# Attention units by head: scores, transposes and values of one head together, values ahead of the hidden-layer tile

## The chip, the cores and the metric

The program runs on one core of one Trainium2 chip. The metric is device time in microseconds of one execution. Engines named below: TensorE (PE in the profile; PEld are its weight loads), VectorE (DVE), ScalarE (ACT), GpSimd (POOL) and SyncE (SP), which issues most of the DMAs.

## The reference

Three stages follow each other. The attention stage has 2 batches, 8 heads, 576 positions and head size 64; half of the heads see the last 32 positions only, the other half see every 32nd position. A mixture of 8 experts over all 1152 rows comes next, and then a mixture in which each row takes its two best experts.

```python
scores = scale * np.matmul(q, k.transpose(0, 1, 3, 2))
mask_local = (rel >= 0) & (rel < stride)
mask_strided = (rel >= 0) & (pos[None, :] % stride == pos[:, None] % stride)
scores = np.where(masks[None, :, :, :], scores, -1000000000.0)
attn = np.exp(scores - np.max(scores, axis=-1, keepdims=True))
attn = attn / (np.sum(attn, axis=-1, keepdims=True) + 1e-09)
x = np.matmul(attn, v)            # rearranged to 1152 x 512
# first mixture: P from x @ w_gate (8 rounds of row and column sums)
for e in range(E):
    out += P[:, e:e + 1] * (np.maximum(x @ w1[e], 0.0) @ w2[e])
# second mixture: the same products, each row with its two best experts only
```

## The kernel before, in words

The change touches the attention stage alone. Its work is cut into 16 units U (`UNITS`); two units make a pair of heads (`g = U // 2`). Units 0 to 3 and 8 to 11 are local (tiles of 96 queries by 128 keys, three per head), units 4 to 7 and 12 to 15 are strided (72 by 72, four per head). In each unit both heads of a pair are worked on: head h=0 has its 64 rows of `qT` and `kT` on partitions 0 to 63, head h=1 on partitions 64 to 127.

There is no scheduler: each engine runs the order written in its block, and semaphores join them. For one unit U the steps are:

- TensorE, `scores(U)` (L1060, L1069): for both heads one matmul that puts the mask into PSUM, then the score matmuls, tile by tile with the two heads taking turns. The mask matmul of head h waits for the exponentials of unit U-1, head h.
- TensorE, `transpose_probs(U - 1, h)` (L1082): the probabilities of the unit before, 0 then 1, each after GpSimd has scaled them (`prs_ready`).
- TensorE, `transpose_half` (L1046): transposes of q or k of the next pair, up to unit 13.
- TensorE, `keep_warm` (L1185): matmuls on zeros without use of their result, one to three a unit in units 3 to 8.
- TensorE, `fill(f)` (L1137 to L1139), units 10 to 15: twelve matmuls of one hidden tile of the first mixture, ahead of `values(U - 1)`. It waits until ScalarE and VectorE have emptied the tile before (`hhi_ready`, `hlo_ready`).
- TensorE, `values(U - 1)` (L1100 local, L1106 strided): probabilities times v, into output partitions 0 to 63 for the one head and 64 to 127 for the other. It waits for both copies of the transposed probabilities (`pT_act` by ScalarE, `pT_dve` by VectorE). After unit 9 the gate logits of batch 0 follow (L1115, L1116).
- VectorE: row maxima of both heads (L764), `hidden_lo` (L745), `x_lo` (L736), `probs_T` (L732), then per head the sum's reciprocal (L780, L781) with q or k copies (L724, L716) and weight splits (L741) behind head 0.
- ScalarE: `x_hi` (L560), `hidden_fill` (L578), `probs_T` (L556), the exponentials (L570), a q copy (L548), weight splits (L505).
- GpSimd: the scaling of the probabilities (L431).

## Time and profile before

| what | us |
|---|---|
| median of 3 executions | 1200.23 |
| the three executions | 1194.28, 1200.35, 1200.23 |
| the profiled execution, its own time | 1194.28 |
| its span in the profile | 1192.5 |
| attention stage in the span (to the last `values`) | 0 to about 104 |
| TensorE busy, whole span | 1165.0 (98%) |

The profile is of the fastest of the three executions. What lies around the span is 1.8 us. The page gives the TensorE clock that was granted in tenths of full speed for 40 slices of the span; its two levels are 2.4 GHz (1.00) and 1.2 GHz (0.50). In the table of stretches further down each row is one unit, cut where its first mask matmul starts. A float32 matmul stands in the trace as two records (16 records for the 8 score matmuls of a strided unit), a transpose or a matmul of the mixtures as one.

### The profile page before, as it was taken

The numbers are of one execution on the slowest core, as the hardware profiler recorded it, in microseconds if no ns is written. First come the engines' busy times: TensorE is split into PE (matmuls) and PEld (weight loads), VectorE is DVE, ScalarE is ACT, GpSimd is POOL, SyncE is SP. The second block draws the span as 40 slices with busy tenths as digits, with TensorE's granted clock in tenths as the row PEclk, the third lists the DMA queues.
The fourth block names the chain that finished last, engine by engine and source line by source line (L and its number), as shares of the span: only waits on it lengthen the run. The fifth ranks groups of instructions, "written<-read, shape, count | busy, mean of one in ns | idle before, by whom it ended". The sixth has DMA issues, their size and how long they took to land.

```text
span 1192.5 us, 19152 instructions
## 1 busy us (share of the span) xinstructions
PE 1165.0 (98%) x6697; PEld 1036.7 (87%) x6697; DVE 486.9 (41%) x1003; ACT 325.2 (27%) x710; POOL 106.7 (9%) x118
## 2 busy tenths in 40 slices
PE   7999999999999999999999999999997999999997
PEld 4677999999999999999999999999896889888885
DVE  4656524213323322411322332241136566665663
ACT  4763113102112211301211221231132334343332
POOL 3222000000000000000000000000001222222221
PEclk9689999999999999999999999999998999999999
DMA  7635104002201200400220220040003666556653
GB/s 167 153 111 163 50 1 137 5 0 70 70 0 57 84 0 0 141 0 0 70 70 0 69 72 0 0 142 27 27 18 103 183 187 178 160 155 166 164 154 79
DMA packets 82337, 96.42 MB, mean 81 GB/s; under 512 B 22176, under 2 KB 56992, under 8 KB 82304
## 3 DMA queue, kind: packets, MB, share of 16 engines
q1 hardware_dynamic: 76400, 81.23, 22.7%
q0 software_dynamic: 5904, 14.75, 5.8%
q8 instruction: 20, 0.33, 0.1%
q14 instruction: 13, 0.11, 0.0%
HBM read 85.05 MB, written 10.91 MB: 80 GB/s over the span
## 4 chain that ended last, share of the span: by engine, by line
PE 95%; DVE 1%; ACT 1%; issue 1%; SPq 1%; DMA 1%; POOL 0%; POOLq 0%; ACTq 0%; DVEq 0%
PE bank L1151 15%; PE bank L1137 15%; PE bank L1153 15%; PE bank L1152 15%; PE bank L1139 14%; PE bank L1138 14%; PE bank L1069 1%; PE bank L1082 1%; PE bank L1358 1%; ACT prs L570 1%; PE bank L1280 1%; PE bank L1060 1%; PE bank L1046 1%; PE bank L1343 1%; PE bank L1185 0%
## 5 line engine op out<-in xcount | busy, mean ns | idle before, releaser
L1151 PE MATMUL bank<-w2hi,hhi 128*128 128x512 f32 (+1 forms) x768 | 301.0, 392 | 0.0
L1153 PE MATMUL bank<-w2hi,hlo 128*128 128x512 f32 (+1 forms) x768 | 299.9, 390 | 0.0
L1152 PE MATMUL bank<-w2lo,hhi 128*128 128x512 f32 (+1 forms) x768 | 299.7, 390 | 0.0
L1137 PE MATMUL bank<-xhi,w1hi 128*128 (+1 forms) x768 | 257.9, 336 | 2.9 <-issue 2.6
L647 ACT ACTIVATE hhi<-bank 128x384 fp32r<-128x384 f32 x184 | 90.5, 492 | 611.8 <-PE bank L1139 611.8
L1139 PE MATMUL bank<-xhi,w1lo 128*128 (+1 forms) x768 | 257.0, 335 | 0.0
L1138 PE MATMUL bank<-xlo,w1hi 128*128 (+1 forms) x768 | 256.8, 334 | 0.0
L745 DVE SCALAR_TENSOR_TENSOR hlo<-bank,hhi 128x384 fp32r<-128x384 f32 (+1 forms) x256 | 139.0, 543 | 265.7 <-ACT hhi L647 234.3
L1153 PEld LDWEIGHTS bank<-w2hi,hlo 128*128 128x128 f32 (+1 forms) x768 | 141.6, 184 | 33.1
L1152 PEld LDWEIGHTS bank<-w2lo,hhi 128*128 128x128 f32 (+1 forms) x768 | 141.7, 184 | 31.0
L1151 PEld LDWEIGHTS bank<-w2hi,hhi 128*128 128x128 f32 (+1 forms) x768 | 141.7, 185 | 30.9
L844 DVE SCALAR_TENSOR_TENSOR acc<-bank,prob,acc 128x512 f32<-128x512 f32 x63 | 47.3, 751 | 266.4 <-PE bank L1153 266.4
L1137 PEld LDWEIGHTS bank<-xhi,w1hi 128*128 128x128 f32 x768 | 144.2, 188 | 4.6 <-issue 3.2
L1138 PEld LDWEIGHTS bank<-xlo,w1hi 128*128 128x128 f32 x768 | 144.2, 188 | 0.9
L1139 PEld LDWEIGHTS bank<-xhi,w1lo 128*128 128x128 f32 x768 | 144.2, 188 | 0.0
L741 DVE TENSOR_TENSOR w2lo<-w2raw,w2hi 128x1024 fp32r<-128x1024 f32 x64 | 78.1, 1221 | 13.7 <-ACT w2hi L505 13.7
L1137 PE MATMUL bank<-x2hi,w1hi 128*128 128x336 f32 x256 | 82.4, 322 | 0.9 <-ACT x2hi L680 0.9
L741 DVE TENSOR_TENSOR w1lo<-w1raw,w1hi 128x1024 fp32r<-128x1024 f32 x68 | 79.9, 1226 | 6.7 <-ACT w1hi L505 6.7
L1139 PE MATMUL bank<-x2hi,w1lo 128*128 128x336 f32 x256 | 81.7, 319 | 0.0
L1138 PE MATMUL bank<-x2lo,w1hi 128*128 128x336 f32 x256 | 81.7, 319 | 0.0
L459 POOL IOTA iotaS<- 128x336 f16 x1 | 0.4, 416 | 749.8 <-PE bank L1139 749.8
L505 ACT ACTIVATE w2hi<-w2raw 128x1024 fp32r<-128x1024 f32 x64 | 67.5, 1054 | 0.0
(176 smaller groups left out, 852.1 us busy)
## 6 DMA issues: line engine op xcount, KB each, us to landing
w1raw<-in_moe_w_dram SPq DMA_DIRECT2D x68, 512.0 KB, 4.6
w2raw<-in_moe_w_dram SPq DMA_DIRECT2D x68, 512.0 KB, 4.3
qkraw<-in_q_dram SPq DMA_DIRECT2D x16, 144.0 KB
qkraw<-in_k_dram SPq DMA_DIRECT2D x16, 144.0 KB
out_dram<-ysb POOLq DMA_DIRECT2D x3, 768.0 KB, 6.4
x1rows<-acc SPq DMA_DIRECT2D x9, 256.0 KB, 2.0
vloc<-in_v_dram SPq DMA_DIRECT2D x8, 144.0 KB
vstr<-in_v_dram SPq DMA_DIRECT2D x8, 144.0 KB
```

Source lines behind the costliest of these rows:

```text
L505: act.activation(hi, raw, ACT.Copy).then_inc(sem_out, 1)
L570: ins = act.activation(prs[0:rows, U % 2, h, t * w:(t + 1) * w], psS[h][0:rows, t * w:(t + 1) * w], ACT.Exp, bias=nmax[0:rows, h, t:t + 1] ...
L647: act.activation(hhi[:, f, :], psH[f % 4][:, 0:GT], ACT.Relu).then_inc(hhi_ready, 1)
L741: dve.tensor_tensor(lo, raw, hi.bitcast(F32), ALU.subtract).then_inc(sem_out, 1)
L745: dve.scalar_tensor_tensor(hlo[:, f, 0:n], bank[:, 0:n], 0.0, hhi[:, f, 0:n].bitcast(F32), ALU.max, ALU.subtract).then_inc(hlo_ready, 1)
L844: dve.scalar_tensor_tensor(acc[:, i, :], psY[i % TT][:, :], w, acc[:, i, :], ALU.mult, ALU.add).then_inc(acc_ready, 1)
L1137: pe.matmul(bank[:, 0:n], wh, xh(c), start=(c == 0), stop=False)
L1138: pe.matmul(bank[:, 0:n], wh, xl(c), start=False, stop=False)
L1139: ins = pe.matmul(bank[:, 0:n], wl, xh(c), start=False, stop=(c == DC - 1))
L1151: pe.matmul(psY[tt][0:rows, :], hh, w2hi[:, f, :], start=(f == 0), stop=False)
L1152: pe.matmul(psY[tt][0:rows, :], hh, w2lo[:, f, :], start=False, stop=False)
L1153: ins = pe.matmul(psY[tt][0:rows, :], hl, w2hi[:, f, :], start=False, stop=(f == FC - 1))
```

## The change

TensorE's `scores` takes the head as an argument: mask and all score matmuls of head 0, then the transposes of head 0 of the unit before, then the same for head 1. In `values` the heads no longer take turns: all tiles of head 0 after a wait for ScalarE's copy, then all of head 1 after a wait for VectorE's. In the strided units the output half is `t // 2`, so there it changes every two matmuls. `values(U - 1)` now stands ahead of `fill(f)`, and the gate logits of batch 0 stay behind the values of their unit. On VectorE `hidden_lo` goes behind `x_lo` and `probs_T`. Nothing changes on ScalarE, GpSimd and SyncE, and no instruction is added or removed.

```diff
--- before.py
+++ after.py
@@ -765,13 +765,13 @@
                                       negate=True).then_inc(max_ready, 1)
                 if U == FILL:
                     sum_parts(0, 0, WHOLE)
-                if U > FILL:
-                    f = U - FILL - 1
-                    hidden_lo(f + 1, f, psF[f])
                 if U >= 2:
                     x_lo(U - 2)
                 if U:
                     probs_T(U - 1)
+                if U > FILL:
+                    f = U - FILL - 1
+                    hidden_lo(f + 1, f, psF[f])
                 for h in range(2):
                     dve.wait_ge(exp_ready, 2 * U + h + 1)
                     if U >= 2:
@@ -1047,31 +1047,28 @@
                                        qkraw[g % 2][:, n, (4 * half + t) * P:(4 * half + t + 1) * P], ident[0:SP_ROWS, 0:SP_ROWS])
                 ins.then_inc(qk_transposed, 1)
 
-            def scores(U):
+            def scores(U, h):
                 g, c, half = U // 2, (U // 2) % PAIRS, U % 2
                 rows, tiles, w = unit_shape(U)
-                pe.wait_ge(qT_act, g + 1)
-                pe.wait_ge(qT_dve, g + 1)
-                pe.wait_ge(kT_ready, 2 * g + 2)
+                if h == 0:
+                    pe.wait_ge(qT_act, g + 1)
+                    pe.wait_ge(qT_dve, g + 1)
+                    pe.wait_ge(kT_ready, 2 * g + 2)
+                if U:
+                    pe.wait_ge(exp_ready, 2 * (U - 1) + h + 1)
                 m = mask_l[:, half, :, :] if c < LOCAL_PAIRS else spread(mask_s[:, :], 1, 4)
-                for h in range(2):
-                    if U:
-                        pe.wait_ge(exp_ready, 2 * (U - 1) + h + 1)
-                    pe.matmul(by(psS[h][0:rows], w, tiles * w), identb[0:rows, 0:rows], m, start=True, stop=False)
+                pe.matmul(by(psS[h][0:rows], w, tiles * w), identb[0:rows, 0:rows], m, start=True, stop=False)
                 for t in range(tiles):
-                    for h in range(2):
-                        if c < LOCAL_PAIRS:
-                            key = query = (half * tiles + t) * rows
-                        else:
-                            head, step, _ = strided_tile(half, h, t)
-                            query = (head * SP_T + step) // 2 * rows
-                            key = STRIDE + query
-                        ins = pe.matmul(psS[h][0:rows, t * w:(t + 1) * w],
-                                        qT[g % 2][h * DH:(h + 1) * DH, query:query + rows],
-                                        kT[g % 2][h * DH:(h + 1) * DH, key:key + w],
-                                        start=False, stop=(t == tiles - 1))
-                        if t == tiles - 1:
-                            ins.then_inc(scores_ready, 1)
+                    if c < LOCAL_PAIRS:
+                        key = query = (half * tiles + t) * rows
+                    else:
+                        head, step, _ = strided_tile(half, h, t)
+                        query = (head * SP_T + step) // 2 * rows
+                        key = STRIDE + query
+                    ins = pe.matmul(psS[h][0:rows, t * w:(t + 1) * w],
+                                    qT[g % 2][h * DH:(h + 1) * DH, query:query + rows],
+                                    kT[g % 2][h * DH:(h + 1) * DH, key:key + w], start=False, stop=(t == tiles - 1))
+                ins.then_inc(scores_ready, 1)
 
             def transpose_probs(U, h):
                 rows, tiles, w = unit_shape(U)
@@ -1092,19 +1089,15 @@
 
                     n_v = sum(6 if j % PAIRS < LOCAL_PAIRS else 2 for j in range(g % 2, g + 1, 2))
                     pe.wait_ge(v_in[g % 2], 16 * n_v)
-                pe.wait_ge(pT_act, U + 1)
-                pe.wait_ge(pT_dve, U + 1)
-                if c < LOCAL_PAIRS:
+                for h in range(2):
+                    pe.wait_ge((pT_act, pT_dve)[h], U + 1)
                     for t in range(tiles):
-                        for h in range(2):
-                            ins = pe.matmul(psO[h * DH:(h + 1) * DH, t * rows:(t + 1) * rows],
-                                            vloc[g % 2][:, h, half * tiles + t, :],
-                                            pT[0:w, h, t * rows:(t + 1) * rows], start=True, stop=True)
-                else:
-                    for h, t in ((0, 0), (1, 2), (0, 1), (1, 3), (1, 0), (0, 2), (1, 1), (0, 3)):
-                        head, step, to = strided_tile(half, h, t)
-                        ins = pe.matmul(psO[head * DH:(head + 1) * DH, to * rows:(to + 1) * rows],
-                                        vstr[g % 2][:, head, step, :],
+                        if c < LOCAL_PAIRS:
+                            head, to, vv = h, t, vloc[g % 2][:, h, half * tiles + t, :]
+                        else:
+                            head, step, to = strided_tile(half, h, t)
+                            vv = vstr[g % 2][:, head, step, :]
+                        ins = pe.matmul(psO[head * DH:(head + 1) * DH, to * rows:(to + 1) * rows], vv,
                                         pT[0:w, h, t * rows:(t + 1) * rows], start=True, stop=True)
                 ins.then_inc(heads_done, 1)
 
@@ -1202,10 +1195,10 @@
                 g = U // 2
                 if U == 2 * LOCAL_PAIRS:
                     pe.wait_ge(mask_s_ready, 1)
-                scores(U)
-                if U:
-                    transpose_probs(U - 1, 0)
-                    transpose_probs(U - 1, 1)
+                for h in range(2):
+                    scores(U, h)
+                    if U:
+                        transpose_probs(U - 1, h)
                 if g + 1 < ALLPAIRS:
 
                     transpose_half(g + 1, U % 2, 0)
@@ -1217,6 +1210,15 @@
                     keep_warm(WARM_FIRST)
                 if WARM_FROM <= U < FILL - 1:
                     keep_warm(WARM_LOCAL if g % PAIRS < LOCAL_PAIRS else WARM_STRIDED)
+                if U:
+                    values(U - 1)
+                if U == FILL - 1:
+
+                    pe.wait_ge(xlo_ready, UNITS // 2)
+                    pe.wait_ge(wgT_zeroed, 1)
+                    pe.wait_ge(wghi_ready, 1)
+                    pe.wait_ge(wglo_ready, 1)
+                    logits(psF[0], 0, WHOLE * P)
                 if U >= FILL:
                     f = U - FILL
 
@@ -1226,15 +1228,6 @@
                     else:
                         pe.wait_ge(lg_copied, 1)
                     fill(f)
-                if U:
-                    values(U - 1)
-                if U == FILL - 1:
-
-                    pe.wait_ge(xlo_ready, UNITS // 2)
-                    pe.wait_ge(wgT_zeroed, 1)
-                    pe.wait_ge(wghi_ready, 1)
-                    pe.wait_ge(wglo_ready, 1)
-                    logits(psF[0], 0, WHOLE * P)
             for h in range(2):
                 transpose_probs(UNITS - 1, h)
             fill(FILLED)
```

TensorE before, from the last hidden-tile matmul of unit 12 to the first of unit 13 (a strided unit; `bank` is PSUM, `vloc` and `vstr` are v):

```order
L1139 MATMUL bank<-xhi,w1lo 128x384
L1100 MATMUL bank<-pT,vloc_93 64x96 x6
L1060 MATMUL bank<-mask_s,identb 72x288 x2
L1069 MATMUL bank<-kT_98,qT_96 72x72 x8
L1082 MATMUL bank<-ident,prs 72x72 x8
L1046 MATMUL bank<-ident,qkraw_91 128x72 x8
L1137 MATMUL bank<-xhi,w1hi 128x384
```

The same place in the changed kernel:

```order
L1132 MATMUL bank<-xhi,w1lo 128x384
L1060 MATMUL bank<-mask_s,identb 72x288
L1068 MATMUL bank<-kT_98,qT_96 72x72 x4
L1079 MATMUL bank<-ident,prs 72x72 x4
L1060 MATMUL bank<-mask_s,identb 72x288
L1068 MATMUL bank<-kT_98,qT_96 72x72 x4
L1079 MATMUL bank<-ident,prs 72x72 x4
L1046 MATMUL bank<-ident,qkraw_91 128x72 x8
L1100 MATMUL bank<-pT,vstr_94 64x72 x8
L1130 MATMUL bank<-xhi,w1hi 128x384
```

The eight score matmuls and eight transposes of a strided unit became two blocks of four and four, and the values moved from behind the twelve hidden-tile matmuls to ahead of them.

VectorE before, at the start of unit 13:

```order
L764 TENSOR_REDUCE nmax<-bank 72x4 x2
L745 SCALAR_TENSOR_TENSOR hlo<-bank,hhi 128x384
L736 TENSOR_TENSOR xlo<-bank,xhi 128x288
L732 COPY pT<-bank 72x288
L780 TENSOR_SCALAR rinv<-rsum 72x4
```

VectorE in the changed kernel, same place:

```order
L764 TENSOR_REDUCE nmax<-bank 72x4 x2
L736 TENSOR_TENSOR xlo<-bank,xhi 128x288
L732 COPY pT<-bank 72x288
L745 SCALAR_TENSOR_TENSOR hlo<-bank,hhi 128x384
L780 TENSOR_SCALAR rinv<-rsum 72x4
```

The rest of the hidden tile moved behind the copy of the transposed probabilities.

## Rows read from the trace of the kernel before

**Rows 1.** The page, the TensorE clock granted in 40 slices.

```profile
PEclk9689999999999999999999999999998999999999
```

**Rows 2.** Busy time by unit: start:end, length, engines (count), clock, DMA share, GB/s.

```profile
20.45:24.34 3.89, 3.12 (x40) 2.45 (x40) 2.36 (x7) 2.13 (x12) 0.96 (x2) 1.00 0.93 296
29.20:33.57 4.37, 3.77 (x48) 2.60 (x48) 2.44 (x10) 2.85 (x18) 1.49 (x2) 1.00 0.88 165
33.57:37.96 4.39, 3.46 (x52) 2.57 (x53) 3.19 (x11) 4.39 (x21) 1.32 (x2) 1.00 0.95 246
37.96:44.04 6.08, 5.48 (x54) 3.76 (x54) 5.17 (x13) 5.59 (x21) 1.50 (x3) 0.63 0.74 169
44.04:50.41 6.37, 6.37 (x56) 4.55 (x55) 3.95 (x9) 4.44 (x19) 1.15 (x2) 0.50 0.45 81
50.41:56.33 5.92, 5.92 (x49) 4.40 (x48) 3.98 (x11) 3.61 (x16) 1.49 (x2) 0.50 0.51 171
56.33:65.63 9.30, 9.25 (x51) 7.10 (x49) 4.91 (x14) 4.54 (x18) 2.47 (x3) 0.50 0.66 165
65.63:72.31 6.68, 6.36 (x58) 5.11 (x57) 3.38 (x10) 4.32 (x16) 1.54 (x2) 0.91 0.00 1
83.63:89.08 5.45, 5.17 (x63) 4.43 (x64) 3.42 (x11) 3.64 (x20) 1.38 (x3) 1.00 0.66 205
```

**Rows 3.** TensorE in order of time: start, length, line; units 12 to 14.

```profile
82.91 0.72 PE L1100 MATMUL bank<-pT,vloc 128*64 128x96 f32 x12
83.56 0.44 PE L1060 MATMUL bank<-mask_s,identb 72*72 72x288 bf16 x2
83.92 0.74 PE L1069 MATMUL bank<-kT,qT 64*72 64x72 f32 x16
84.60 0.69 PE L1082 MATMUL bank<-ident,prs 72*72 72x72 f32 x8
85.13 0.67 PE L1046 MATMUL bank<-ident,qkraw 72*128 72x72 f32 x8
86.08 0.41 PE L1137 MATMUL bank<-xhi,w1hi 128*128 128x384 f32 x1 [0.28 <-issue]
...
88.36 0.72 PE L1106 MATMUL bank<-pT,vstr 72*64 72x72 f32 x16
...
91.53 0.41 PE L1137 MATMUL bank<-xhi,w1hi 128*128 128x384 f32 x1 [0.79 <-issue]
```

**Rows 4.** TensorE in order of time, one lone float32 matmul at full clock.

```profile
114.00 0.34 PE L1161 MATMUL bank<-prob,ones 128*128 128x72 f32 x2
114.14 0.48 PE L1151 MATMUL bank<-w2hi,hhi 128*128 128x512 f32 x1
```

**Rows 5.** TensorE in order of time, a local unit at full clock.

```profile
72.70 0.90 PE L1069 MATMUL bank<-kT,qT 64*96 64x128 f32 x12
73.53 0.71 PE L1082 MATMUL bank<-ident,prs 96*128 96x96 f32 x6
74.08 0.67 PE L1046 MATMUL bank<-ident,qkraw 72*128 72x72 f32 x8
```

**Rows 6.** TensorE in order of time, a strided unit at half clock.

```profile
44.67 1.24 PE L1069 MATMUL bank<-kT,qT 64*72 64x72 f32 x16
45.84 1.17 PE L1082 MATMUL bank<-ident,prs 72*72 72x72 f32 x8
```

**Rows 7.** VectorE in order of time, behind the score matmuls of unit 12.

```profile
79.28 0.82 DVE L764 TENSOR_REDUCE nmax<-bank 72x4 f32<-72x288 f32 x2 [1.96 <-PE bank L1069]
80.02 0.54 DVE L745 SCALAR_TENSOR_TENSOR hlo<-bank,hhi 128x384 fp32r<-128x384 f32 x1
...
80.84 0.44 DVE L732 COPY pT<-bank 128x288 f32<-128x288 f32 x1
```

**Rows 8.** TensorE in order of time, the waits ahead of the clock's fall.

```profile
37.96 0.41 PE L1060 MATMUL bank<-mask_s,identb 72*72 72x288 bf16 x2 [0.92 <-ACT prs L570]
...
40.01 0.70 PE L1082 MATMUL bank<-ident,prs 72*72 72x72 f32 x4 [0.60 <-POOL prs L431]
```

## The prediction

> **What bounds the kernel now.** I read the page first. TensorE is busy nearly all the time, but its clock is not at full speed everywhere [rows 1]: slices 2 and 3 and a stretch from about 40 to 67 us. The change touches only the first 104 us, so I cut that part into units [rows 2]. Three kinds show. Early units at full clock (unit 2 of 3.89 us, unit 5 of 4.39) leave TensorE idle 0.77 and 0.93 us; what ends the idle time is the softmax chain, as in unit 6, where the mask matmul waits 0.92 us for ScalarE's exponentials and the transposes 0.60 us for GpSimd [rows 8]. Units 6 to 9 run at clock 0.50 and are TensorE throughout: 6.37 busy of 6.37 us in unit 7. Unit 6 has a mean clock of 0.63, so 0.74 x 6.08 = 4.5 us of it are at half speed and the fall is at 39.5 us; unit 10 has 0.91, so the full clock is back 1.2 us into it, at 66.8. Units 10 to 15 are TensorE again, at full clock: in unit 13 5.17 of 5.45 us are busy, the rest is 0.28 us ahead of the hidden tile; without q and k transposes (units 14, 15) that wait is 0.79 [rows 3].
>
> So the change is worth what it does to TensorE's own work from unit 6 on; a shorter softmax chain can earn only in units 1 to 5.
>
> **Part 1: the heads no longer take turns.** The 16 score records of a strided unit take 84.60 - 83.92 = 0.68 us, 0.042 each, with 72 columns a record. The transposes beside them, also 72 columns a record but without turns, take 85.13 - 84.60 = 0.53 for 8, 0.066 each [rows 3]. A lone float32 matmul of 72 columns takes 0.14 us for its two records, 0.070 each [rows 4]. I read this as the two heads, on different halves of the partitions, running side by side. Bounds: if a score record never gained from its neighbour, the change costs nothing here; if each costs 0.070, a unit's scores take 1.12 instead of 0.68, +0.44. I take 0.066, the nearest row: 16 x 0.066 = 1.06, +0.38. Local: 96-column transposes take (74.08 - 73.53) / 6 = 0.092, so 128 columns 0.122, 12 x 0.122 = 1.47 instead of 73.53 - 72.70 = 0.83: +0.64 [rows 5]. Values alternate between output halves and show the same price: local 12 records in 83.56 - 82.91 = 0.65 us; alone 12 x 0.092 = 1.10, +0.45. Strided values are as long (0.72 busy in both rows); the half still changes three times in eight matmuls, which saves about three of 16 records: 13 x 0.066 = 0.86, +0.21 [rows 3].
>
> The Trainium skill's page "TensorEngine Tiling (Array Packing)", section "Theoretical Speedup", gives up to 2x for a small dimension of 64 or less. By it a strided unit's scores would go from 0.68 to at most 1.36, +0.68 instead of my +0.38; the rows are nearer to 1.6x with the turnarounds inside, and the sum goes by them.
>
> **Part 2: more turnarounds.** Per unit there is one more passage from transposes to mask and one more from mask to scores. The two mask matmuls start 0.36 us ahead of the scores, and 2 x 288 columns at 2.4 GHz are 0.24, so a passage costs 0.12 [rows 3]. Two more: +0.25 us a unit (bounds 0 and 0.4, the latter if the passages scores to transposes count too).
>
> **Part 3: values ahead of the hidden tile.** In units 10 to 15 values now wait for VectorE's copy: from the end of the scores 0.1 to the maximum, 0.37 for the second maximum (0.74 for two, from 79.28 to 80.02), 0.36 for x_lo, 0.44 for the copy: 1.3 us [rows 7]. TensorE meanwhile has the second transposes (0.27) and q and k transposes (0.5): a wait of 0.5 us in units 10 to 13, 1.0 in 14 and 15. Queued behind it are the hidden tile and the next unit's scores. The wait for the emptied hidden bank goes: VectorE's part of it, 0.5 us after the copy, ends while the values run. So 0.5 takes the place of 0.28 and 1.0 that of 0.79: +0.2 a unit, six units, +1.2 (bounds 0 and +3). I take +1.0, since the last transposes of unit 15 come later in the order and wait less.
>
> **Part 4: the head start of the softmax.** Head 0's scores no longer wait for head 1's exponentials, but VectorE's maximum still stands behind its reciprocal of head 1, and ScalarE's exponentials behind the probability copy. It helps units with idle TensorE only. New queueing: head 1's scores now stand behind head 0's transposes, which wait for GpSimd's scaling; TensorE reaches them late enough to hide it.
>
> **The sum**, against the profiled execution's own 1194.28 us (span 1192.5):
> - Units 0 to 5: unit 2 gets 0.64 + 0.45 + 0.25 = 1.34 us of work for 0.77 of idle: +0.6. Unit 4 gets 0.38 + 0.45 + 0.25 = 1.08 for 0.60: +0.5. Unit 5 gets 0.84 for 0.93: 0. The others about 0. Total +1.
> - Units 6 to 9, if the clock stays low there. At half clock scores show 45.84 - 44.67 = 1.17 us against 0.68 [rows 6], and I double the extra records. Unit 7: 0.76 + 0.45 + 0.3 = +1.5. Unit 8: local scores 1.28 + 0.45 + 0.3 = +2.0. Unit 9: 1.28 + 0.9 + 0.3 = +2.5. Unit 6: 1.4 less the 0.60 wait: +0.8. Total +6.8.
> - Units 10 to 15 at full clock: units 10 and 11 1.34 each, unit 12 1.08, units 13 to 15 0.84 each, last values 0.21: 6.5, and Part 3's 1.0: +7.5.
>
> 1 + 6.8 + 7.5 = 15.3, so 1194.28 + 15.3 = 1209.6. The forecast is 1210. The median before is 1200.23, 6 us over the profiled execution; what those 6 us are the trace can't show. The sum stands on the profiled one, and the top of the range allows for them.
>
> **The rivals.**
> - *B, the clock stays up.* The fall at 39.5 comes after waits of 0.92 and 0.60 us [rows 8]; the change fills such gaps. Then units 6 and 7 would take about 4.6 each (unit 5's 4.39 and a little), unit 8 4.6, unit 9 4.9 plus logits at full clock 1.75: 20.5 instead of 27.67, -7.2; with +1 and +7.5 the time is 1195.6 (1201.6 with the 6 us above). For it: less idle. Against it: 25 us of gapless work in units 6 to 9 did not bring the clock back; it returned only after the eight full-width logits matmuls. The skill's page "TensorE: Matmul & The Clock Gate", section "HAM oscillation", blames idle gaps longer than any here; by it the clock would have held in the kernel before as well. The trace disagrees (0.92 us was the longest gap near the fall), so the page doesn't move the chance.
> - *C, taking turns bought nothing, and the change is faster.* Place: the score and value records. If their 0.042 us is what a record costs in any order, TensorE gains only the turnarounds, 16 x 0.25 = 4 us, half of them in idle time; the earlier exponentials close the 0.77 and 0.93 us gaps (-2), and the clock holds (units 6 to 9 19.1 us, -8.6). 1194.28 - 8.6 - 2 + 2 is about 1186. It decides if four head-0 score matmuls take under 0.4 us. Against it: [rows 4] and the transposes.
> - *D, the half clock reaches past the logits* into unit 10, since the matmuls on both sides of them are now narrower for longer. Unit 10 has about 7.9 us of work; 5 more: 1215.
>
> **Chances.** Forecast 0.56, B 0.22, C 0.12, D 0.10. Under 0.5% a measurement of this kernel can't be told from no change: three executions differ by 6 us. Faster by more (below 1194.2): C and a sliver of B, 0.13. Within: B, 0.21. Slower (above 1206.2): forecast and D, 0.66. The range reaches from under B to over D, 1193 to 1217; the forecast's own is 1205 to 1216.
>
> **What would show it.** Four head-0 score matmuls at full clock: 0.5 us of start-to-start, or 0.35 if C holds. Unit 13 about 6.5 us instead of 5.45, with a wait of about 0.5 ahead of the values and none ahead of the hidden tile. Clock 0.50 between about 40 and 74 us. If that stretch is missing, B holds and units 10 to 15 must still be 7 us longer. If units 10 to 15 are no longer than before, Part 1 is wrong.

## The result, and the profile after

| what | before | after |
|---|---|---|
| median, us | 1194.53 (20 executions) | 1206.02 (20) |
| lowest to highest | 1186.21 to 1203.68 | 1193.36 to 1226.87 |
| the profiled execution, its own time | 1194.28 | 1205.9 |
| its span | 1192.5 | 1204.1 |

The ratio after to before is 1.0074, 95% interval 1.0045 to 1.0103: slower, by 0.7%. The comparison leaves out executions more than 1.5% above the fastest of their kernel, so the longest ones of the changed kernel (1219.75 to 1226.87 us) are in its median and not in the ratio.

The page of the changed kernel, the TensorE clock granted in 40 slices (compare [rows 1]):

```profile
PEclk9788999999999999999999999999998999999999
```

Busy time by stretch, with columns as in [rows 2]: units 7, 8, 9, 10 and 13, then units 0 to 9, units 10 to 13, and unit 14 to the first output matmul behind the hidden tiles.

```profile
42.33:49.01 6.68, 6.00 (x56) 4.45 (x54) 6.21 (x15) 5.58 (x21) 1.73 (x4) 0.68 0.64 120
49.01:56.71 7.70, 7.70 (x50) 5.78 (x48) 3.64 (x8) 3.88 (x16) 1.46 (x2) 0.50 0.41 135
56.71:67.97 11.26, 11.26 (x50) 8.70 (x49) 4.65 (x14) 4.65 (x16) 2.47 (x3) 0.50 0.48 137
67.97:75.96 7.99, 7.31 (x57) 6.02 (x56) 3.47 (x10) 4.83 (x17) 1.65 (x2) 0.95 0.13 34
88.96:95.02 6.06, 6.00 (x63) 5.11 (x62) 3.36 (x11) 3.93 (x19) 1.33 (x2) 1.00 0.93 293
9.97:67.97 58.00, 55.24 (x445) 41.85 (x451) 35.59 (x97) 37.88 (x165) 15.35 (x21) 0.80 0.68 166
67.97:95.02 27.05, 26.20 (x227) 22.07 (x226) 13.90 (x42) 17.93 (x73) 5.96 (x8) 0.99 0.35 107
95.02:118.49 23.47, 21.94 (x174) 19.74 (x172) 12.83 (x27) 10.88 (x44) 3.56 (x4) 0.85 0.25 65
```

The same three long stretches of the kernel before:

```profile
9.35:65.63 56.28, 49.22 (x451) 35.28 (x451) 34.90 (x97) 36.82 (x165) 15.31 (x21) 0.74 0.72 173
65.63:89.01 23.38, 22.05 (x228) 18.36 (x226) 13.47 (x42) 16.92 (x72) 5.86 (x8) 0.97 0.27 83
89.01:108.58 19.57, 17.45 (x176) 15.42 (x174) 12.41 (x27) 11.07 (x45) 3.58 (x5) 1.00 0.43 128
```

The spans differ by 11.6 us: 0.6 ahead of unit 0, 58.00 - 56.28 = 1.7 in units 0 to 9, 27.05 - 23.38 = 3.7 in units 10 to 13, 23.47 - 19.57 = 3.9 behind them, and the remaining 1.7 after the attention stage, where the changed kernel has a bit at lower clock (0.86 from 860 to 872 us) and the one before none (1.00). In units 0 to 9 TensorE is busy 6.0 us more (55.24 against 49.22) in 1.7 us more time, and this although the kernel before spent more of its time there at half clock (mean 0.74 against 0.80): idle time takes up the difference. In units 10 to 13 it is busy 4.15 us more, and 3.7 show; behind them it is busy 4.49 more, and 3.9 show.

TensorE in order of time (start, length, line): the longest wait near the clock's fall, a local unit, the strided unit 13 at full clock, and the values of unit 14 with what follows; last, VectorE's copy of the transposed probabilities that unit 13's values need. To be read against [rows 3], [rows 5] and [rows 8]:

```profile
44.93 0.70 PE L1079 MATMUL bank<-ident,prs 72*72 72x72 f32 x4 [0.46 <-POOL prs L431]
...
76.22 0.89 PE L1068 MATMUL bank<-kT,qT 64*96 64x128 f32 x6
77.04 0.47 PE L1079 MATMUL bank<-ident,prs 96*128 96x96 f32 x3
...
79.50 1.07 PE L1100 MATMUL bank<-pT,vloc 128*64 128x96 f32 x12
80.51 0.44 PE L1130 MATMUL bank<-xhi,w1hi 128*128 128x384 f32 x1
...
88.96 0.29 PE L1060 MATMUL bank<-mask_s,identb 72*72 72x288 bf16 x1
89.18 0.73 PE L1068 MATMUL bank<-kT,qT 64*72 64x72 f32 x8
89.84 0.44 PE L1079 MATMUL bank<-ident,prs 72*72 72x72 f32 x4
90.12 0.29 PE L1060 MATMUL bank<-mask_s,identb 72*72 72x288 bf16 x1
90.34 0.73 PE L1068 MATMUL bank<-kT,qT 64*72 64x72 f32 x8
91.01 0.45 PE L1079 MATMUL bank<-ident,prs 72*72 72x72 f32 x4
91.29 0.67 PE L1046 MATMUL bank<-ident,qkraw 72*128 72x72 f32 x8
91.99 0.84 PE L1100 MATMUL bank<-pT,vstr 72*64 72x72 f32 x16
92.86 0.41 PE L1130 MATMUL bank<-xhi,w1hi 128*128 128x384 f32 x1
93.46 0.33 PE L1130 MATMUL bank<-xhi,w1hi 128*128 128x384 f32 x1
93.98 0.33 PE L1130 MATMUL bank<-xhi,w1hi 128*128 128x384 f32 x1
...
98.26 0.83 PE L1100 MATMUL bank<-pT,vstr 72*64 72x72 f32 x16 [0.75 <-DVE xlo L736]
99.98 0.52 PE L1130 MATMUL bank<-xhi,w1hi 128*128 128x384 f32 x1
100.94 0.52 PE L1130 MATMUL bank<-xhi,w1hi 128*128 128x384 f32 x1
...
91.85 0.44 DVE L732 COPY pT<-bank 72x288 f32<-72x288 f32 x1
```

Take the differences of starts. One head's eight strided score records last 89.84 - 89.18 = 0.66 us, the other's 0.67: 1.33 for both, where the sixteen took 0.68 by turns [rows 3]. Locally one head takes 77.04 - 76.22 = 0.82, two 1.65, against 0.83 for both [rows 5]. So a head alone takes as long as both took together. The single records of the trace show how. A strided head's eight records start 0.12 us after each other once and then every 0.065 us, and 0.155 passes from the last to the next transposes: 0.66. That is so for head 0 alone, and it is so by turns, where head 1's records start 0.006 us behind head 0's. The transposes next to them are as before (0.28 for four, 0.53 for eight). From one block's transposes to the mask and on to the scores nothing stands idle: the mask matmul takes 90.34 - 90.12 = 0.22 us, of which 288 columns at 2.4 GHz are 0.12.

### The profile page after: what moved, and what is told of

Same layout as the page of the kernel before. It is cut to its first block, busy times and chain, and to the rows that moved or that the text cites. A ratio compares the mean times of both kernels' runs of the same rounds, so it can differ in the third digit from the quotient of the medians.

```text
span 1204.1 us, 19140 instructions
## 1 busy us (share of the span) xinstructions
PE 1182.2 (98%) x6692; PEld 1053.3 (87%) x6697; DVE 488.6 (41%) x1003; ACT 327.3 (27%) x710; POOL 107.0 (9%) x118
## 4 chain that ended last, share of the span: by engine, by line
PE 96%; DVE 2%; issue 1%; DMA 0%; ACT 0%; POOLq 0%; POOL 0%; DVEq 0%
PE bank L1130 15%; PE bank L1144 15%; PE bank L1146 15%; PE bank L1145 15%; PE bank L1131 14%; PE bank L1132 14%; PE bank L1068 2%; PE bank L1100 1%; PE bank L1079 1%; PE bank L1351 1%; PE bank L1178 1%; PE bank L1273 1%; PE bank L1336 1%; PE bank L1060 1%; PE bank L1046 1%
```

## The experiments

The question was which part costs the time, and by what. The first theory: two heads' score matmuls, on different halves of the partitions, run side by side while they stand next to each other, and the change ends that. Its rivals: the order of the values or their place ahead of the hidden tile costs it; turns help only since neighbours write to different banks of PSUM; or the clock alone makes the difference.

Times vary between executions of one kernel, and the reason is in every record: the mean granted clock. With two levels, 1.00 and 0.50, the time spent at the lower is 2 x (1 - mean clock) x span. The mean is given in thousandths, so this time comes in steps of 2.4 us. Over 37 executions of the changed kernel the time follows it closely: 21 us of half clock gave 1193.3 us, 36 gave 1200, 51 gave 1205 to 1206, 58 gave 1208, 105 gave 1227, about 0.39 us for each. The kernel before, over 29 executions on one chip: 17 us gave 1186.3, 43 gave 1194.4, 53 gave 1196.7, 65 gave 1199.5, about 0.28 each. At equal half-clock time the changed kernel is 6 to 7 us longer at 21, about 9 at 43 to 46, and 10 to 11 at 53. It is therefore slower by its own work, and half clock adds to it.

### One part at a time

**Scores and transposes by head, nothing else.**

```diff
-                scores(U)
-                if U:
-                    transpose_probs(U - 1, 0)
-                    transpose_probs(U - 1, 1)
+                for h in range(2):
+                    scores(U, h)
+                    if U:
+                        transpose_probs(U - 1, h)
```

> The kernel before with one part of the change: mask, scores and transposes of one head together; values still take turns and stand behind the hidden tile. Theory S (the two heads' score matmuls, on different partition halves, ran side by side, and that is lost): one head's scores take 0.67 us strided and 0.83 local, as long as both heads' before; units 11 to 13, at full clock, 0.8 to 1.3 us longer each than 5.90, 5.42, 5.45; 5 to 9 us more in the median. Theory F (what costs is the values' new place, with its wait and the clock's later falls): at most 3 us more.

Measured: median 1215.32 us (6 executions, 1204.56 to 1218.42) against 1194.34; ratio 1.0172 (1.0123 to 1.0221). The stretch from 20 to 80 us:

```profile
20.00:80.00 60.00, 58.92 (x368) 44.31 (x371) 30.27 (x81) 32.84 (x138) 11.59 (x16) 0.50 0.46 130
```

Theory S put it 5 to 9 us above the kernel before, and it came out 21 above. This part alone is slower than the whole change, and its profiled execution ran at half clock for all of these 60 us, with TensorE busy 58.92 of them; the full clock came back at 80.9, in the middle of the full-width logits matmuls. Its six executions had 51 to 88 us at half clock, and the one with 51 took 1204.56, where the full change with as much takes 1205 to 1206. So the scores carry the loss; what is worse here than in the full change is the clock.

**Values head after head, nothing else** (the loop of the changed kernel in `values`, in its old place).

```diff
-                pe.wait_ge(pT_act, U + 1)
-                pe.wait_ge(pT_dve, U + 1)
...
+                for h in range(2):
+                    pe.wait_ge((pT_act, pT_dve)[h], U + 1)
...
-                    for h, t in ((0, 0), (1, 2), (0, 1), (1, 3), (1, 0), (0, 2), (1, 1), (0, 3)):
```

> The kernel before with one part of the change: in the values all tiles of head 0, then all of head 1, with a wait for each. Theory S: local values take 1.0 us from start to next start instead of 0.65, strided ones about 0.7; 8 local units times 0.35, part of it in idle time: 1 to 3 us more. My prediction's size (0.45 and 0.21 a unit): 3 to 5 us. Theory F: nothing, within 1 us.

Measured: 1193.06, ratio 0.9997 (0.9964 to 1.0031). No difference, though theory S had expected 1 to 3 us. TensorE in order of time, local values and what follows them:

```profile
81.99 0.93 PE L1103 MATMUL bank<-pT,vloc 128*64 128x96 f32 x12
82.85 0.44 PE L1060 MATMUL bank<-mask_s,identb 72*72 72x288 bf16 x2
```

Here, where both copies have long been made, local values take 82.85 - 81.99 = 0.86 us against 0.65 by turns [rows 3], and head 1's first record starts 0.22 us behind head 0's. Strided ones take 88.33 - 87.63 = 0.70 against 0.65.

**Values ahead of the hidden tile, nothing else** (the two calls exchanged on TensorE, and `hidden_lo` moved on VectorE).

```diff
-                if U >= FILL:
-                    f = U - FILL
...
-                    fill(f)
                 if U:
                     values(U - 1)
...
+                    fill(f)
```

> The kernel before with one part of the change: values ahead of the hidden tile, and VectorE's rest of the hidden tile behind its probability copy. Theory S: the wait ahead of the hidden tile (0.28, in units 14 and 15 0.79 us) is replaced by one of about 0.3 to 0.5 (1.0) ahead of the values: between -1 and +2 us. Theory F: 4 us or more slower, with the clock at half in units 14 and 15 as in the changed kernel.

Measured: 1194.62, ratio 1.0011 (0.9979 to 1.0042). No difference. TensorE in order of time, the values of two units:

```profile
86.23 0.72 PE L1106 MATMUL bank<-pT,vstr 72*64 72x72 f32 x16 [0.59 <-DVE pT L732]
...
92.09 0.72 PE L1106 MATMUL bank<-pT,vstr 72*64 72x72 f32 x16 [1.31 <-DVE pT L732]
```

Here the waits of Part 3 stand about as it put them: 0.59 in unit 13 and 1.31 in unit 14, for VectorE's copy. They take the place of the 0.28 and 0.79 ahead of the hidden tile [rows 3] and cost next to nothing. In the full change they are shorter: none is listed in unit 13 (the values at 91.99 stand right behind the q and k transposes, from 91.29), and in unit 14 it is 0.75 and ends with `x_lo`. The next experiment shows why.

**Both value parts, scores as before.**

> The changed kernel with the scores and transposes back as before: both heads' score matmuls by turns; values in order and ahead of the hidden tile stay. Theory S: 1 to 4 us more than before, so most of the change's cost is gone. Theory F: as slow as the changed kernel, 8 us or more over before.

The edit is the two above together. Measured: 1194.38, ratio 0.9997 (0.9961 to 1.0032). Its profiled execution (1185.53 us) held the full clock throughout the attention stage; units 0 to 9, and unit 13:

```profile
9.32:56.34 47.02, 38.09 (x446) 28.21 (x452) 35.18 (x97) 36.43 (x165) 15.31 (x21) 1.00 0.82 198
74.62:80.01 5.39, 5.22 (x63) 4.56 (x62) 3.42 (x11) 4.12 (x21) 1.20 (x2) 1.00 0.93 292
```

The values of units 13 and 14 in that execution:

```profile
76.97 0.84 PE L1103 MATMUL bank<-pT,vstr 72*64 72x72 f32 x16
...
82.58 0.83 PE L1103 MATMUL bank<-pT,vstr 72*64 72x72 f32 x16 [0.86 <-DVE xlo L736]
```

The scores are as before here, and still unit 13 has no listed wait (0.14 us in the trace) and unit 14 one of 0.86 instead of 1.31. So it is not longer scores that shorten the waits: with the values in order head 0 needs only ScalarE's copy and the emptied output bank (`x_lo`), and only head 1 waits for VectorE's copy, which comes 0.36 us after `x_lo`. Part of that wait has moved in between the two heads' values, where no idle time is listed. In the changed kernel's unit 13 the copy ends at 91.85 + 0.44 = 92.29 and head 1's first value record starts at 92.35, 0.36 us behind head 0's; strided values take 92.86 - 91.99 = 0.87 us there against 0.70 without the wait.

Unit 13 takes 5.39 us against 5.45 before [rows 2]. Everything but the scores is neutral to within 0.4%.

### Why a head alone takes as long as two

**Turns of two matmuls instead of one.**

```diff
-                for t in range(tiles):
-                    for h in range(2):
+                for t0 in range(0, tiles, 2):
+                    for h, t in [(h, t) for h in range(2) for t in range(t0, min(t0 + 2, tiles))]:
```

> The kernel before, but the heads' score matmuls take turns by two tiles instead of one (head 0 tiles 0 and 1, head 1 tiles 0 and 1, and so on). Theory L (the matmuls of the two partition halves are two streams, and the later one starts a few matmuls ahead of its turn): strided scores stay at 0.67 to 0.75 us at full clock, as with single turns. Rival (only direct neighbours overlap): a strided unit has 3 changes of half instead of 7, and its scores take about 1.0 us.

Measured, one execution: 1187.95 us with 24 us at half clock; the kernel before took 1187.94 and 1187.99 with as much on that chip. TensorE in order of time:

```profile
77.55 0.80 PE L1069 MATMUL bank<-kT,qT 64*72 64x72 f32 x16
78.28 0.69 PE L1082 MATMUL bank<-ident,prs 72*72 72x72 f32 x8
```

The sixteen records take 0.73 us instead of 0.68. Two matmuls of one head in a row still run beside the other head's: strict turns are not needed, only nearness.

**Transposes by turns.** If turns helped because neighbours write to different banks, the probability transposes of the two heads (banks `psP[0]` and `psP[1]`, all on the same partitions from 0) would gain as well.

```diff
+                for t in range(tiles):
+                    for h in range(2):
+                        ins = pe.transpose(psP[h][0:w, t * rows:(t + 1) * rows],
+                                           prs[0:rows, U % 2, h, t * w:(t + 1) * w], ident[0:rows, 0:rows])
```

> The kernel before, but the transposes of the probabilities take turns between the two heads: other PSUM bank each time, same partitions 0 to 71 or 0 to 95 each time. Theory H (it is the partition half that lets score matmuls run side by side): transposes stay at 0.066 us (strided) and 0.092 us (local) each, 0.53 and 0.55 for a unit. Rival (turns between PSUM banks are what helps): they fall towards half, 0.3 us.

Measured, one execution: 1198.77 us at a mean clock of 0.975, so its time says nothing. TensorE in order of time:

```profile
87.27 0.69 PE L1094 MATMUL bank<-ident,prs 72*72 72x72 f32 x8
87.80 0.67 PE L1046 MATMUL bank<-ident,qkraw 72*128 72x72 f32 x8
```

The transposes take 87.80 - 87.27 = 0.53 us, as without turns [rows 3]. For transposes on the same partitions, different banks give nothing. The values show the other side: both heads' values go to one bank (`psO`), into different halves of its partitions, and they do run side by side (0.65 us by turns against 0.86 one head after the other). Whether scores on two input halves would overlap in one bank no run shows.

**Heads in blocks, nothing between them.** All score matmuls of head 0, then all of head 1, masks ahead of both and transposes behind.

```diff
-                for t in range(tiles):
-                    for h in range(2):
+                for h in range(2):
+                    for t in range(tiles):
```

> The kernel before, both masks first, then all score matmuls of head 0, then all of head 1, nothing between the two blocks. Theory L (a matmul of the free half starts up to about two matmuls ahead of its turn, as head 1 did in the changed kernel's local values): a strided unit's 16 records take 0.9 to 1.0 us at full clock, between 0.68 by turns and 1.33 with the transposes between; a local unit's 1.1 to 1.4. Rival N (what stops the overlap in the change is what stands between the heads, mask and transposes over all partitions, and nothing else): 0.68 to 0.75 as by turns. Rival O (no looking ahead at all): 1.1 or more.

Measured: 1202.15 us (9 executions) against 1195.07, ratio 1.0092 (1.0059 to 1.0126). TensorE in order of time, a local and a strided unit:

```profile
77.98 1.19 PE L1069 MATMUL bank<-kT,qT 64*96 64x128 f32 x12
79.11 0.71 PE L1082 MATMUL bank<-ident,prs 96*128 96x96 f32 x6
...
83.78 1.06 PE L1069 MATMUL bank<-kT,qT 64*72 64x72 f32 x16
84.77 0.71 PE L1082 MATMUL bank<-ident,prs 96*128 96x96 f32 x6
```

Strided scores take 0.99 us, between 0.68 by turns and 1.33 with transposes between; local ones 1.13, between 0.83 and 1.65. In the trace head 1's first record starts 0.32 us into the block, beside head 0's fifth: the last two matmuls of head 0 run beside the first two of head 1, and no more. From its first record on head 1 then takes its 0.67 us as alone: 0.32 + 0.67 = 0.99. So TensorE starts a matmul of the other half up to about two matmuls ahead of its turn. In the changed kernel transposes and the mask, which use partitions of both halves, stand between the blocks, and nothing is side by side. Those are five matmuls in a strided unit, more than the two that could be overtaken in any case; so no run tells whether it is their number or their use of both halves that keeps the heads apart.

### The clock held by wide matmuls

The rival "it is the clock" needs kernels whose clock does not differ. In the kernel before the clock came back behind the eight full-width logits matmuls, so this edit puts two more 128 x 512 matmuls behind the values of each of units 3 to 9, and two in each of units 14 and 15 where there are no q and k transposes. (These are 18; the expectation below counts 16.) Their results are not used.

```diff
+                if g + 1 >= ALLPAIRS:
+                    for i in range(2):
+                        pe.matmul(psX[1][:, :], w1hi[:, 0, 0:P], w1hi[:, 0, 0:512], start=True, stop=True)
...
                 if U:
                     values(U - 1)
+                if WARM_FROM <= U < FILL:
+                    keep_warm(2)
```

**The changed kernel with it:**

> The changed kernel with more matmuls without use of their result (128 rows, 512 columns): two behind the values of units 3 to 9, two ahead of the values in units 14 and 15. Theory K (the change's cost is 5 to 7 us of matmul time, and the rest is time at half clock that its denser row of narrow matmuls brings): the half clock between 40 and 70 us and in units 14 and 15 is gone, the time is 1188 to 1193 and hardly varies. If the clock is not to be held by this: 1207 or more, since the added work is 16 x 0.21 = 3 us.

**The kernel before with it:**

> The kernel before with the same added wide matmuls. Theory K: the added ones lie mostly in idle time (0.8 to 0.9 us a unit), the half clock is gone, and the time is 1182 to 1187 instead of 1194, hardly varying; the distance to the changed kernel with the same addition is then the change's matmul time alone, 5 to 7 us. Without a hold on the clock: 1194 to 1197.

Measured on one chip: changed 1195.28 (12 executions, nine of them 1193.63 to 1195.52), ratio 1.0055 (1.0018 to 1.0091); before 1186.19 (1183.8 to 1190.77), ratio 0.9972 (0.9946 to 0.9998), both against the plain kernel before. The clock rows of the changed one and of the one before:

```profile
PEclk9999999999999999999999999999998999999999
```

```profile
PEclk8999999999999999999999999999998999999999
```

The changed kernel's median falls from 1206 to 1195.3 with 14 to 19 us left at half clock in those nine, and it stays 1195.28 - 1186.19 = 9.1 us above the kernel before with the same edit. Both theory K's 1188 to 1193 and its distance of 5 to 7 us were too low. So of the 11.5 us between the two medians some 9 are the change's own work, and 2 to 3 that it spends more time at half clock: 51 us in its commonest executions against 43 in the median one of the kernel before. The means lie further apart, 59 us over 37 executions against 38 over 29. In the profiles of both kernels and of all five with wide matmuls 6 to 13 us of the half clock lie between 800 and 960 us, which the change does not touch; so only part of the 14 to 19 us left is in the attention stage.

**Scores by head alone, with it; and values and hidden tile alone, with it:**

> Mask, scores and transposes of one head together, nothing else of the change, with the added wide matmuls. Theory S (at a clock that is held, the whole change's cost is the lost side-by-side of the scores): about 1195, 8 to 10 us over the kernel before with the same addition (1186.2). Rival M (the parts work on each other, and without the values' move the scores' part costs more, as 1215 without the addition may suggest): 1200 or more.

> Values in order and ahead of the hidden tile, VectorE's order as changed, scores of both heads by turns as before, with the added wide matmuls. Theory S: 1185 to 1188, like the kernel before with the addition. Rival M: 1190 or more.

**The kernel before, with wide matmuls from unit 1 on** (`1 <= U < FILL` for `WARM_FROM <= U < FILL`):

> The kernel before with the added wide matmuls behind the values from unit 1 on instead of from unit 3. Theory K: the half clock that was still there between 20 and 31 us goes too, 1183 to 1186 and with less spread. Rival: in units 1 and 2 the added 0.43 us lie on the path that the key copies set, and 2 x 0.43 us are lost: 1187.

Measured on one chip, ratios to the plain kernel before (1194.53): scores alone 1199.59, 1.0039 (1.0003 to 1.0076); values and hidden tile alone 1187.38, 0.9933 (0.9897 to 0.9969); wide matmuls from unit 1 1186.76, 0.994 (0.9905 to 0.9975). The usual execution of "scores alone" still had 31 us at half clock; its two with 17 and 19 us took 1194.5 and 1194.8, as the whole change does with wide matmuls (1195.3). So at an equal clock the scores account for all of it, by these two executions; the median of "scores alone", 1199.59, lies between theory S's 1195 and rival M's 1200. Values and hidden tile alone came out as theory S had it. Wide matmuls from unit 1 on gained nothing over those from unit 3: 1186.76 is the rival's 1187, not theory K's 1183 to 1186.

The profiled executions of two of these held clock 1.00 through all of the attention stage, so their tables of stretches show the lost side-by-side by itself. The kernel before with wide matmuls from unit 1; units 0 to 9, unit 10 to the first output matmul, unit 13:

```profile
9.67:57.06 47.39, 39.98 (x461) 27.80 (x469) 35.10 (x97) 36.37 (x165) 15.35 (x21) 1.00 0.78 187
57.06:99.57 42.51, 40.06 (x404) 34.09 (x403) 25.92 (x69) 28.05 (x117) 9.46 (x12) 1.00 0.42 123
74.45:79.90 5.45, 5.17 (x64) 4.43 (x62) 3.42 (x11) 3.72 (x20) 1.36 (x3) 1.00 0.65 207
```

Scores by head with wide matmuls, the same stretches:

```profile
9.47:60.80 51.33, 46.47 (x458) 33.93 (x465) 35.56 (x97) 37.74 (x165) 15.32 (x21) 1.00 0.75 180
60.80:107.50 46.70, 45.21 (x404) 38.06 (x403) 26.88 (x69) 28.26 (x117) 9.50 (x12) 1.00 0.36 106
80.64:86.76 6.12, 5.94 (x64) 5.06 (x62) 3.36 (x11) 3.59 (x19) 1.33 (x2) 1.00 0.72 218
```

In units 0 to 9 TensorE works 6.5 us more and ends 3.9 us later, since 2.6 us fall into idle time; from unit 10 on it works 5.2 us more and ends 4.2 later. Together 8.1 us (the kernel before carries four wide matmuls more, in units 1 and 2, so this is rather too little), and unit 13 is 0.67 us longer, which is the 1.33 - 0.68 = 0.65 of its scores.

What stays open: why the scores by head alone spend more time at half clock than the whole change does (51 to 88 us in six executions, and 31 against 17 to 19 with wide matmuls). The whole change also moves the values, which alone cost nothing. That was not taken further.

The kernels that beat both are the one before with wide matmuls, from unit 1 (ratio 0.994), from unit 3 (0.9972), or with the values' part of the change (0.9933). Each gains under 1%, and which of the three is best is not settled: the first and last ran on one chip and overlap, and the second was set against a kernel before that happened to run at 1187.96 there. What they all do is make the time steady: 1183.8 to 1191 us, where the kernel before spreads from 1186 to 1203.

## Why the prediction was right, and where its terms were off

The forecast was 1210 us, slower, with an own range of 1205 to 1216. The median is 1206.02 and the profiled execution 1205.9. The mechanism was Part 1's and it held. Some terms were mis-sized, and that the total fits is partly luck: against the profiled execution the sum is 3.7 us too large (15.3 for 11.6), made of 1.5 too much in units 0 to 5, 4.5 too much in units 6 to 9, nothing in units 10 to 15 for two errors that cancel, and 2.3 us outside of the attention units that no term has. The median lies only 1 us inside the own range, while single executions run from 1193 to 1227 us with their time at half clock. The 6 us by which the median of three (1200.23) stood over the profiled execution, which the prediction left open, are of that kind too: over 20 executions that median is 1194.53.

- **Part 1, scores, and Part 2, turnarounds: right together, wrongly split.** Part 1 took +0.38 us for strided scores and +0.64 for local ones. Measured: 1.33 - 0.68 = +0.65, and 1.65 - 0.83 = +0.82. The record time of 0.066 was right (0.065 in the trace; locally 0.109 for 0.122). The mis-sized step is what goes with it: Part 1 set 16 bare record times against a measured 0.68 that holds a head's slower first step and the passage to the transposes, together 0.15 us, and the changed kernel pays these 0.15 twice: 16 x 0.065 + 2 x 0.145 = 1.33. Part 2 meant such passages, +0.25 a unit, but at the masks: those, now apart, take 0.22 us each where the pair took 0.36 [rows 3], +0.1. Both parts together gave +0.63 and +0.89, and the rows give +0.73 and +0.88. The Trainium skill's page "TensorEngine Tiling (Array Packing)", section "Theoretical Speedup", gives up to 2x for 64 rows or less. The trace agrees with it (1.33 / 0.68 = 1.96); its +0.68 with Part 2's +0.25 on top would have been 0.93, further off.
- **Part 1, values: about right in size, partly for another cause.** Local values take 80.51 - 79.50 = 1.01 us against 0.65, +0.36 for the +0.45 expected; strided ones 0.87 against 0.65, +0.22 for +0.21. But the order alone costs +0.21 and +0.05, as the values in order show (0.86 and 0.70); the rest is head 1's wait for VectorE's copy, which Part 3 had ahead of all values. Head 1's first local value records still run beside head 0's last.
- **Part 3, waits: the step that failed in units 10 to 15.** It put 0.5 us ahead of the values in units 10 to 13 and 1.0 in 14 and 15, and +1.0 in all. The trace lists 0.68 in unit 10, none in 11 to 13 and 0.75 in 14 and 15, all for `x_lo`: head 0 of the values does not wait for VectorE's copy at all. From unit 10 on TensorE is idle 0.85 + 1.53 = 2.4 us against 1.33 + 2.12 = 3.45 before (length less busy time in the three long stretches): 1.1 less instead of 1.0 more. Where both copies are waited for, the waits were 0.59 and 1.31, and still neutral.
- **Part 4 and units 0 to 5.** Expected +1 us, measured 28.08 against 28.61: -0.5. Of that the kernel before owes some to a bit of half clock of its own, from 12.2 to 15.6 us, which the changed one's profiled execution lacks.
- **Units 6 to 9: expected +6.8, measured 67.97 - 38.05 = 29.92 against 27.67, +2.3.** Unit 8 took 7.70 against 5.92, +1.8 for +2.0; unit 9 11.26 against 9.30, +2.0 for +2.5. These hold. The miss is in units 6 and 7: the clock fell at 44.8, not at 39.5, so unit 6 ran at full clock (4.28 us instead of 6.08). The sum had held the fall where it was. So 3.8 us of the forecast hung on where the clock falls, and that differs between executions.
- **Units 10 to 15: expected +7.5, measured 50.52 - 42.95 = +7.6, for other reasons.** TensorE is busy 4.15 + 4.49 = 8.6 us more and idle 1.1 less; the sum had 6.5 and 1.0 more idle. Unit 13 took 6.06, not 6.5 us. In units 14 and 15 the clock fell twice, as the table of stretches shows:

```profile
44.80:68.70 23.90, 23.55 (x127) 17.59 (x129) 12.15 (x31) 12.13 (x49) 4.70 (x7) 0.50 0.45 123
99.40:102.80 3.40, 3.40 (x12) 3.32 (x11) 0.17 (x1) 0.46 (x1) 1.29 (x2) 0.50 0.00 0
106.20:109.65 3.45, 3.45 (x24) 3.31 (x25) 3.37 (x8) 1.51 (x7) 2.27 (x2) 0.51 0.00 0
```

  There three hidden-tile matmuls take 0.96 us (starts at 99.98 and 100.94) and at full clock 0.52 (93.46 and 93.98), so 6.9 us at half clock cost about 6.9 x (1 - 0.52 / 0.96) = 3. Neither the sum nor a rival had this. Without it units 10 to 15 would be about 4.5 us longer than before, not 7.5; the clean pair says 4.2 for the scores alone. So the agreement here is luck. The falls follow waits of 0.75 us, but the kernel before has 0.79 in the same units [rows 3] and "both value parts" 0.86, both without a fall; what brings it is open.
- **Rival B, the clock stays up,** is not what usually happens, but it does happen: the executions with 21 us of half clock took 1193.3 us, near its 1195.6. The sum took half clock as either there or not; it is a spread of 21 to 105 us in the same kernel.
- **Rival C, turns bought nothing,** is refuted: four head-0 score matmuls take 0.66 us, above the 0.4 from which it decided, and the kernels without side-by-side scores are 8 to 9 us longer at equal clock.
- **Rival D, half clock past the logits,** did not come: unit 10 has clock 0.95, before 0.91 [rows 2]. Where the executions with over 70 us at half clock have it is open, since none of them was profiled.

That the loss is the scores' own work is shown by the clean pair of profiles (8.1 us at clock 1.00) and by the value experiments, which moved nothing. Not shown is why the change has more half clock in its usual executions.

## What to carry to other kernels

Matmuls on disjoint halves of the partitions (64 rows each) overlapped here only while they stood within about two matmuls of each other in the order; keep them adjacent, and put masks and transposes ahead of or behind the pair, not between. When a block is priced by its record time, add the slower first step and the passage behind it, once for each block. When a kernel's time spreads by more than the effect looked for, take the mean granted clock of each execution, turn it into time at half clock, and compare executions of equal half-clock time before blaming the change. A few wide matmuls in a narrow stretch can be worth more than their own time.

## What the runs showed of the hardware

- Two streams of float32 matmuls on different partition halves run fully side by side (0.68 us for both, 0.66 for one), and nearly so in turns of two (0.73). In blocks of four only two matmuls of each overlap (0.99). With transposes and a mask between them nothing does (1.33).
- A float32 score record of 72 columns starts 0.065 us after the one before; the first step of a block takes 0.12, and 0.155 passes from its last record to the transposes.
- Two heads' values overlap though they write one PSUM bank, in different halves of its partitions (0.65 us by turns, 0.86 one after the other); transposes on the same partitions that alternate between two banks do not (0.53, as without turns).
- One kernel's executions differ by where the half clock falls: 17 to 77 us of it in the kernel before (1186 to 1203 us), 21 to 105 in the changed one (1193 to 1227). Each microsecond of it costs 0.28 and 0.39 us. 23.55 of 23.90 busy us in the changed kernel, and 58.92 of 60.00 with the scores alone, passed at half clock; in both it ended in or behind the full-width logits matmuls, as in the kernel before. With heads in blocks a first stretch at half clock ended at 36.4 us, in the last of three wide matmuls.
- The changed kernel's main fall of the clock, at 44.8 us, lies in a wait of 0.46 us, with nothing longer in the unit ahead of it, and the one at 99.4 behind a wait of 0.75; waits of 0.79 and 0.86 elsewhere were followed by none. The Trainium skill's page "TensorE: Matmul & The Clock Gate", section "HAM oscillation", blames longer idle gaps; none as long as it names stands near these falls.
